# Second attention unit: own buffer for moved x, earlier transpose of routing weights, GpSimd's first weight splits between key products

## The chip, the cores and the metric

The kernel runs on one core of a Trainium2 chip. The metric is the device time of one launch in microseconds; the times shown are of whole launches, and one launch was also profiled. Engines are called by their short names: PE (TensorE), PEld (its weight loads), DVE (VectorE), ACT (ScalarE), POOL (GpSimd), SP (SyncE, which here only issues DMAs).

## The reference, cut to what matters

```python
def _attn_ref(q, k, v, alpha):            # (4, 8, 768, 48)
    for t in range(S):
        state = alpha[:, :, t, :, None] * state + np.einsum('bhd,bhe->bhde', k[:, :, t], v[:, :, t])
        y[:, :, t] = np.einsum('bhd,bhde->bhe', q[:, :, t], state)

def _moe_ref(x, domain_probs, w1, w2):    # N 3072, D 384, E 4, F 1024
    p = domain_probs / (domain_probs.sum(-1, keepdims=True) + 1e-09)
    for e in range(E):
        h = np.maximum(x @ w1[e], 0.0)
        out += p[:, e:e + 1] * (h @ w2[e])

def _moe2_ref(x, w_in, w_out):            # 384 -> 2048 -> 384
    h = x @ w_in
    g = h - np.tanh(h)
    return (g @ w_out).astype(np.float32)

attn_out = _attn_ref(**attn_kwargs)
x = attn_out.transpose(0, 2, 1, 3).reshape(B * S, H * D)
x = _moe_ref(x=x, **moe_kwargs)
return _moe2_ref(x=x, **moe2_kwargs)
```

## The kernel before, in words

**Units and blocks.** The gated attention is computed in twelve units of 256 tokens (three per batch row, each in chunks of 64 tokens). The two dense stages work on six blocks of 512 tokens, two units each. A matmul of the dense stages is done three times, on a rounded high part and a low rest of each operand, which ACT rounds and DVE or POOL subtracts. Block 0 needs units 0 and 1; these two are computed in a prologue, and the other ten are woven into the dense loops, a step of a unit at a time (`units_at`). Units 0 and 1 have two separate sets of tiles; a name with a b at its end (`R2b`, `KUb`, `SCb`) belongs to unit 1.

**The order** on every engine is written out by hand, one stream per engine, and engines wait on semaphores. Ahead of the loop over blocks the streams hold, per unit:

- PE: `diagonal` (L508) and `scores` (L530) are products of keys and queries at three levels; `turn` (L543) transposes the keys; `deltas` (L554) is keys times values of a chunk; `attend` (L567) gives the unit's outputs, in two halves, `attend(u, 0)` and `attend(u, 1)`. In between stands one transpose of the routing weights `prob` (L688). The first product of the dense stage, `first(0, 0)` (L611 to L613), waits for x of both units.
- DVE: `rotate` (L931 to L939, with `distant`, L296 and L300) scales queries for the next level; `pick` (L912) copies wanted scores out of PSUM under a mask from SBUF into `SC`; `states` (L956, L965, L969) carries the state over the four chunks, `state = fade * state + delta`; `probabilities` (L1089 to L1098) normalises the routing weights; `low_x` (L975 to L980) subtracts for the low part of x.
- ACT: `lay` (L751) lays out the turned keys, `join` (L735 to L741) puts scores and queries together, `carry` (L764, L770) copies states next to the values, `high_x` (L779 to L782) rounds x to its high part. Before `carry(0)` ACT copies the transposed routing weights to `PT` (L850).
- POOL: `raise_keys` (L1198) scales the keys, `tabulate` (L1174) makes tables of decay products, `split_low` (L1209) makes the low rest of one slot of weights; `prepare(2)` (L1174, L1184, L296, L300) is unit 2's table and query work.
- SP: loads; then `move(0)` and `move(1)` (L354), six small DMAs each, which bring the rows that `high_x` and `low_x` left in the tile `XS` to their places in the block's x tile `XB`; and behind them the loads of further weights.

**What orders the work near the change.** There is one tile `XS`. `high_x(u)` waits ahead of its first write until all six DMAs of `move(u - 1)` have landed (L778). PE's stream is `scores(1, 2, 1)`, `turn(1, 0)`, `turn(1, 1)`, the transpose of `prob`, `attend(0, 0)`, and so on. ACT's stream there is `join(0)`, the copy to `PT`, `carry(0)`, `lay(1, 0)`, `lay(1, 1)`, `join(1)`, `high_x(0)`, `carry(1)`, `high_x(1)`. `join(1)` waits for all picks of unit 1 and its last `rotate`. DVE's stream there is `probabilities`, `states(0)`, `pick(1, 2, 0)`, `rotate(1, 2)`, `pick(1, 2, 1)`, `states(1)`, `low_x(0)`, `low_x(1)`. POOL's stream has the four first splits behind `raise_keys(1, 2)` and a wait for `rotate(1, 2)`, and `prepare(2)` behind them.

Of the kernel before, what the change touches and what calls it, by code (L numbers as in the profile page):

```python
# [7 lines left out]
fp32 = mybir.dt.float32  # L8
f32r = mybir.dt.float32r
i32 = mybir.dt.int32  # L10
ALU = mybir.AluOpType
ACT = mybir.ActivationFunctionType
# [3 lines left out]
E, DM, F, F2 = 4, 384, 1024, 2048  # L16
N = B * S
P = 128
CH = 64
# [4 lines left out]
SPARE = P // 2 - D  # L24
TB = 512
NTB = N // TB
TT = TB // P
# [4 lines left out]
UT = 256  # L32
# [20 lines left out]
LEAD = 4  # L53
# [32 lines left out]
def own(u):  # L86

    return int(u == 1)
# [6 lines left out]
def turn_of(u):  # L95

    return len(same_set(u))
# [47 lines left out]
def program(nc, qka_d, v_d, dp_d, w1_d, w2_d, win_d, wout_d, mask_d, ones_d, ident_d, out_d):  # L145
    ctx = ExitStack()
    with ctx:
# [5 lines left out]
        def place(name, words, dt=fp32):  # L153
            offset[name] = at[0]
            at[0] += (4 * words + 31) // 32 * 32
            assert at[0] <= nc.sbuf_usable_end, name
            return nc.alloc_sbuf_tensor_at(name, [P, words], dt, offset=offset[name])
# [6 lines left out]
        ident = place("ident", P)  # L164
# [26 lines left out]
        TOTALS = sum(SPAN) // 4 * 5 + sum(SPAN[1:])  # L191
        TOT = [place("TOT", TOTALS), lend("TOTb", TOTALS, "XB1", 2 * KT * TB, UW)]
        T64 = [place(f"T64_{n}", CHUNKS) for n in range(2)]
        XS = place("XS", 2 * UT, f32r)

        scratch_d = nc.dram_tensor("scratch", (SLOTS, P, RW), fp32, kind="Internal").ap()
        probs_d = nc.dram_tensor("probs", (E * NTB * TT, P), fp32, kind="Internal").ap()
# [105 lines left out]
        def fill_bank(u, k):  # L303
            return bank[RING_ALONE * u + k % RING_ALONE] if u < AHEAD else a_bank[k % 2]
# [30 lines left out]
        def _(sp):  # L335
# [12 lines left out]
            def move(u):  # L348
                for j in (2, 0, 1):
                    sp.wait_ge(x_low[own(u)], 3 * turn_of(u) + (2 if j == 2 else 3))  # L350
                    for hh in range(2):
                        src = XS[CH * hh + SPARE * j:CH * hh + SPARE * (j + 1), :].rearrange("p (h t) -> p h t", h=2)
                        dst = x_tile(u)[CH * hh + D:CH * hh + CH, :, j, x_tokens(u)]
                        sp.dma_start(dst.bitcast(fp32), src.bitcast(fp32)).then_inc(moved[own(u)], 16)  # L354

# [116 lines left out]
        def _(pe):  # L472
# [63 lines left out]
            def turn(u, n):  # L536
                if u == 0:
                    pe.wait_ge(ident_in, 16)
                pe.wait_ge(keys_up[own(u)], 3 * turn_of(u) + 3)
                bank_free(u, 14 + n)  # L540
                for m in range(4):
                    c = (4 * n + m) * P
                    last = nc.tensor.transpose(fill_bank(u, 14 + n)[:, m * P:m * P + P], KU[own(u)][:, c:c + P], ident[:, :])  # L543
                last.then_inc(filled[own(u)], 1)
# [137 lines left out]
            deltas(0, 1)  # L682
            scores(1, 2, 0)
            scores(1, 2, 1)
            turn(1, 0)
            turn(1, 1)
            pe.wait_ge(prob_step, E + 2)
            nc.tensor.transpose(bank[3][0:E * NTB * TT, 0:P], prob[:, :], ident[:, :]).then_inc(prob_turned, 1)  # L688
            attend(0, 0)
            pe.wait_ge(prob_laid, 1)  # L690
            attend(0, 1)
# [30 lines left out]
        def _(act):  # L722
# [49 lines left out]
            def high_x(u):  # L772
                x, t = x_tile(u), x_tokens(u)
                if u // 2 >= 2:
                    act.wait_ge(hid, SLOTS * (u // 2 - 1))
                act.wait_ge(filled[own(u)], filled_at(u, 18))
                if u:
                    act.wait_ge(moved[own(u - 1)], 96 * turn_of(u - 1) + 96)  # L778
                nc.scalar.activation(XS[:, 0:UT], fill_bank(u, 18)[:, UT:2 * UT], ACT.Copy).then_inc(x_high[own(u)], 1)  # L779
                nc.scalar.activation(x[:, 0, 2, t], fill_bank(u, 18)[:, 0:UT], ACT.Copy).then_inc(x_high[own(u)], 1)  # L780
                act.wait_ge(filled[own(u)], filled_at(u, 19))
                nc.scalar.activation(x[:, 0, 0:2, t], fill_bank(u, 19)[:, :].rearrange("p (a t) -> p a t", a=2),  # L782
                                     ACT.Copy).then_inc(x_high[own(u)], 1)
# [95 lines left out]
        def _(dve):  # L879
# [92 lines left out]
            def low_x(u):  # L972
                x, t = x_tile(u), x_tokens(u)
                dve.wait_ge(x_high[own(u)], 3 * turn_of(u) + 2)
                nc.vector.tensor_tensor(XS[:, UT:2 * UT], fill_bank(u, 18)[:, UT:2 * UT], XS[:, 0:UT].bitcast(fp32),  # L975
                                        ALU.subtract).then_inc(x_low[own(u)], 1)
                nc.vector.tensor_tensor(x[:, 1, 2, t], fill_bank(u, 18)[:, 0:UT], x[:, 0, 2, t].bitcast(fp32),
                                        ALU.subtract).then_inc(x_low[own(u)], 1)
                dve.wait_ge(x_high[own(u)], 3 * turn_of(u) + 3)
                nc.vector.tensor_tensor(x[:, 1, 0:2, t], fill_bank(u, 19)[:, :].rearrange("p (a t) -> p a t", a=2),  # L980
                                        x[:, 0, 0:2, t].bitcast(fp32), ALU.subtract).then_inc(x_low[own(u)], 1)
# [178 lines left out]
        @block.gpsimd  # L1160
        def _(pool):
            def tabulate(u, first=0, last=9):
                n = 9 * turn_of(u)
                for i in range(first, last):
                    t, two, three = tables(u, i // 3)
                    if i:
                        pool.wait_ge(tabled[own(u)], n + i)
                    if i % 3 == 0:
                        out, a, b = two, t[:, :, 0:3], t[:, :, 1:4]
                    elif i % 3 == 1:  # L1170
                        out, a, b = three, two[:, :, 0:2], t[:, :, 2:4]
                    else:
                        out, a, b = total(u, i // 3 + 1).rearrange("p (n a) -> p n a", a=1), three[:, :, 0:1], t[:, :, 3:4]
                    nc.gpsimd.tensor_tensor(out, a, b, ALU.mult).then_inc(tabled[own(u)], 1)  # L1174

            def prepare(u):
                n = turn_of(u)
                pool.wait_ge(a_in[own(u)], 16 * (n + 1))
                pool.wait_ge(rotated[own(u)], 3 * n)
                pool.wait_ge(keys_up[own(u)], 3 * n)  # L1180
                pool.wait_ge(stated[own(u - 2)], stated_at(u - 2, states_in(u - 2)))
                tabulate(u, 0, 1)
                pool.wait_ge(q_in[own(u)], 16 * (n + 1))
                nc.gpsimd.tensor_tensor(queries(u, 0, 0, 4), R1[own(u)][:, 0:UW].rearrange("p (n b) -> p n b", b=4),  # L1184
                                        tables(u, 0)[0], ALU.mult).then_inc(spread[own(u)], 1)
                pool.wait_ge(spread[own(u)], 2 * n + 1)
                pool.wait_ge(tabled[own(u)], 9 * n + 1)
                distant(nc.gpsimd, u, 0).then_inc(spread[own(u)], 1)
                tabulate(u, 1, 9)

            def raise_keys(u, level):
                h = LEVELS[level]
                pool.wait_ge(filled[own(u)], filled_at(u, 5 + 4 * level))
                pool.wait_ge(tabled[own(u)], 9 * turn_of(u) + 3 * level + 2)
                t, two, three = tables(u, level)
                for sub, x in ((0, three[:, :, 1:2]), (1, two[:, :, 2:3]), (2, t[:, :, 3:4])):
                    k = blocks(KU[own(u)][:, :], h)[:, :, sub, :]
                    last = nc.gpsimd.tensor_tensor(k, k, x.to_broadcast([P, UW // (4 * h), h]), ALU.mult)  # L1198
                last.then_inc(keys_up[own(u)], 1)

            def attention(u, step):
                if step in (3, 6, 9):
                    raise_keys(u, step // 3 - 1)
                if step == 13 and follower(u) is not None:
                    prepare(follower(u))

            def split_low(g):
                pool.wait_ge(w_high, g + 1)
                nc.gpsimd.tensor_tensor(ring_split(g, 1), WS[g % STAGES][:, :].rearrange("p (w c) -> p w c", w=2),  # L1209
                                        ring_split(g, 0).bitcast(fp32), ALU.subtract).then_inc(w_low, 1)  # L1210

            pool.wait_ge(a_in[1], 16)
            tabulate(1, 0, 1)
            raise_keys(0, 0)
            tabulate(1, 1, 9)
            raise_keys(0, 1)
            raise_keys(1, 0)
            raise_keys(0, 2)
            raise_keys(1, 1)
            raise_keys(1, 2)  # L1220
            pool.wait_ge(rotated[1], 3)
            for g in range(LEAD):
                split_low(g)
            prepare(2)
            for m in range(NTB):
                for s in range(SLOTS1):
                    for u, step in units_at(m, s):
                        attention(u, step)
                    if m == 0:
                        split_low(s + LEAD)  # L1230
# [38 lines left out]
```

## Time and profile before

| what | value |
|---|---|
| time, median of 3 runs | 1415.84 us (1415.15 to 1416.24) |
| the profiled execution's own time | 1413.88 us |
| its span, first to last instruction | 1412.0 us |
| busy share of the span: PE / PEld / DVE / ACT / POOL | 96% / 80% / 62% / 40% / 20% |
| mean granted TensorE clock | 0.984 of full speed |
| the same in the first five of 40 slices of the span | 0.9, 0.6, 0.7, 0.9, 0.9 |
| chain that ended last, by engine | PE 87%, DVE 9%, issue 2%, ACT 1%, DMA 1% |

A slice is 35.3 us. PE's busy share is 0.3, 0.5, 0.5 in the first three slices and 0.9 in all later ones. A granted clock of 1.0 is 2.4 GHz, 0.5 is 1.2 GHz.

### The profile page before, as it was taken

How to read it: one execution, taken by the hardware profiler on the slowest of the kernel's cores; microseconds unless marked ns; L12 is line 12 of the kernel's file. 1: busy time of each engine (PE TensorE's matmuls, PEld its weight loads, DVE VectorE, ACT ScalarE, POOL GpSimd, SP SyncE). 2: the span in 40 equal slices, each digit the busy share in tenths (PEclk: the TensorE clock that was granted, in tenths of full speed). 3: DMA queues.
4: the chain of work that ended last, by engine and by line, in shares of the span. 5: the costliest groups of instructions: out<-in, count | busy, mean ns of one | idle time of the engine just before them, and what ended most of it. 6: DMA issues, size and time to landing. Idle time of an engine off the chain costs nothing.

```text
span 1412.0 us, 25677 instructions
## 1 busy us (share of the span) xinstructions
PE 1352.7 (96%) x10177; PEld 1133.5 (80%) x10177; DVE 877.8 (62%) x1676; ACT 561.2 (40%) x1004; POOL 281.1 (20%) x277
## 2 busy tenths in 40 slices
PE   3559999999999999999999999999999999999999
PEld 3447878887878898888898787888787889888888
DVE  9856574896465686554587455487546468423386
ACT  1414325861313662222474321475131366211175
POOL 4645766001313001304000312300131000000000
PEclk9679999999999999999999999999999999999999
DMA  7258697976565655655655665565656465655552
GB/s 218 69 188 294 220 304 249 335 276 209 175 209 198 236 185 177 221 186 197 224 209 167 227 203 187 194 235 180 209 176 194 167 214 187 209 193 193 181 201 88
DMA packets 104966, 289.06 MB, mean 205 GB/s; under 512 B 10032, under 2 KB 64912, under 8 KB 104848
## 3 DMA queue, kind: packets, MB, share of 16 engines
q1 hardware_dynamic: 104848, 287.43, 60.3%
q8 instruction: 81, 1.33, 0.4%
q14 instruction: 37, 0.30, 0.1%
HBM read 242.52 MB, written 42.52 MB: 202 GB/s over the span
## 4 chain that ended last, share of the span: by engine, by line
PE 87%; DVE 9%; issue 2%; ACT 1%; DMA 1%; SPq 0%; DVEq 0%; ACTq 0%
PE bank L611 14%; PE bank L612 13%; PE bank L613 13%; PE bank L635 9%; PE bank L637 9%; PE bank L636 9%; PE bank L661 4%; PE bank L659 4%; PE bank L660 4%; PE bank L530 3%; PE bank L567 2%; PE bank L554 1%; DVE SC L912 1%; PE bank L508 1%; PE bank L543 1%
## 5 line engine op out<-in xcount | busy, mean ns | idle before, releaser
L809 ACT ACTIVATE HH<-GG 128x512 fp32r<-128x512 f32 x192 | 121.2, 631 | 664.4 <-PE bank L637 529.5
L611 PE MATMUL bank<-XB,RG 128*128 128x512 f32 x864 | 349.6, 405 | 10.1 <-DMA XB<-XS 9.8
L612 PE MATMUL bank<-XB,RG 128*128 128x512 f32 x864 | 340.2, 394 | 0.0
L613 PE MATMUL bank<-XB,RG 128*128 128x512 f32 x864 | 339.2, 393 | 0.0
L1013 DVE SCALAR_TENSOR_TENSOR GG<-bank,PB 128x512 f32<-128x512 f32 x192 | 133.3, 694 | 326.0 <-PE bank L613 325.7
L635 PE MATMUL bank<-HH,RG 128*128 128x512 f32 x576 | 224.7, 390 | 1.5 <-ACT OUT L842 1.5
L636 PE MATMUL bank<-HH,RG 128*128 128x512 f32 x576 | 224.3, 389 | 0.0
L637 PE MATMUL bank<-HL,RG 128*128 128x512 f32 x576 | 224.2, 389 | 0.0
L1198 POOL TENSOR_TENSOR KU<-KU,TOT 128x256 f32<-128x256 f32 x88 | 68.9, 809 | 704.2 <-PE bank L530 704.2
L611 PEld LDWEIGHTS bank<-XB,RG 128*128 128x128 f32 x864 | 162.7, 188 | 50.9 <-issue 10.1
L613 PEld LDWEIGHTS bank<-XB,RG 128*128 128x128 f32 x864 | 162.7, 188 | 35.6
L612 PEld LDWEIGHTS bank<-XB,RG 128*128 128x128 f32 x864 | 162.9, 189 | 28.8
L1019 DVE TENSOR_TENSOR HL<-GG,HH 128x512 fp32r<-128x512 f32 x192 | 157.8, 822 | 8.8 <-ACT HH L809 8.8
L912 DVE COPY_PREDICATED SC<-masks,bank 128x192 f32<-128x192 int32 (+2 forms) x396 | 99.1, 358 | 69.5 <-PE bank L530 69.3
L661 PE MATMUL bank<-RG,HL 128*128 128x384 f32 x384 | 129.5, 337 | 0.0
L659 PE MATMUL bank<-RG,HH 128*128 128x384 f32 x384 | 129.3, 337 | 0.0
L635 PEld LDWEIGHTS bank<-HH,RG 128*128 128x128 f32 x576 | 108.1, 188 | 26.3 <-issue 3.6
L660 PE MATMUL bank<-RG,HH 128*128 128x384 f32 x384 | 128.9, 336 | 0.0
L637 PEld LDWEIGHTS bank<-HL,RG 128*128 128x128 f32 x576 | 108.1, 188 | 22.8
L636 PEld LDWEIGHTS bank<-HH,RG 128*128 128x128 f32 x576 | 108.1, 188 | 22.5
L1036 DVE TENSOR_TENSOR GG<-SQ,bank 128x512 f32<-128x512 f32 x96 | 65.6, 683 | 39.2 <-ACT TH L819 39.2
L818 ACT ACTIVATE SQ<-bank 128x512 f32<-128x512 f32 x96 | 57.2, 596 | 67.6 <-PE bank L613 67.6
(127 smaller groups left out, 1684.1 us busy)
## 6 DMA issues: line engine op xcount, KB each, us to landing
RG<-scratch SPq DMA_DIRECT2D x240, 768.0 KB, 4.3
scratch<-RG SPq DMA_DIRECT2D x48, 768.0 KB, 5.1
VS<-vp SPq DMA_DIRECT2D x11, 768.0 KB, 5.9
WS<-w SPq DMA_DIRECT2D x32, 192.0 KB, 3.3
PB<-probs SPq DMA_DIRECT2D x6, 1024.0 KB, 7.2
AU<-qka SPq DMA_DIRECT2D x11, 512.0 KB, 5.4
R<-qka SPq DMA_DIRECT2D x11, 512.0 KB, 5.3
KU<-qka SPq DMA_DIRECT2D x11, 512.0 KB, 5.8
```

The source lines that it names most:

```text
L611: nc.tensor.matmul(out, w1(g, 0, kt), x_part(m, 0, kt), start=(kt == 0), stop=False)
L612: nc.tensor.matmul(out, w1(g, 0, kt), x_part(m, 1, kt), start=False, stop=False)
L613: last = nc.tensor.matmul(out, w1(g, 1, kt), x_part(m, 0, kt), start=False, stop=(kt == KT - 1))
L635: nc.tensor.matmul(out, w2(g, 0)[:, c], HH[:, h_slot(g)], start=(s == 0), stop=False)
L636: nc.tensor.matmul(out, w2(g, 1)[:, c], HH[:, h_slot(g)], start=False, stop=False)
L637: return nc.tensor.matmul(out, w2(g, 0)[:, c], HL[:, h_slot(g)], start=False, stop=(s == SLOTS1 - 1))
L659: nc.tensor.matmul(out, HH[:, h], w2(g, 0), start=(f == 0), stop=False)
L660: nc.tensor.matmul(out, HH[:, h], w2(g, 1), start=False, stop=False)
L661: last = nc.tensor.matmul(out, HL[:, h], w2(g, 0), start=False, stop=(f == SLOTS2 - 1))
L809: nc.scalar.activation(HH[:, h_slot(g)], GG[:, h_slot(g)], ACT.Copy).then_inc(high, 1)
L1013: nc.vector.scalar_tensor_tensor(GG[:, h_slot(g)], h_bank[s % 2][:, :], 0.0, PB[:, e * TB:e * TB + TB], op0=ALU.max, op1=ALU.mult).then_in ...
L1019: nc.vector.tensor_tensor(HL[:, h_slot(g)], GG[:, h_slot(g)], HH[:, h_slot(g)].bitcast(fp32), ALU.subtract).then_inc(low, 1)
```

## The change

`XS` becomes a pair of tiles, one per set, so that unit 1 writes `XSb`; the wait ahead of `high_x` is now for the last move out of the same tile, which unit 1 has none of. On PE the transpose of `prob`, with its wait for `probabilities`, goes ahead of `turn(1, 0)`. On POOL the first two splits go ahead of `raise_keys(1, 1)`, behind a wait for the first `queries_up` of unit 1 (which `rotate(1, 0)` gives), the third stands between `raise_keys(1, 1)` and `raise_keys(1, 2)`, the fourth behind it; the wait for `rotate(1, 2)` is gone.

```diff
-        XS = place("XS", 2 * UT, f32r)
+        XS = [place("XS", 2 * UT, f32r), place("XSb", 2 * UT, f32r)]
...
-                        src = XS[CH * hh + SPARE * j:CH * hh + SPARE * (j + 1), :].rearrange("p (h t) -> p h t", h=2)
+                        src = XS[own(u)][CH * hh + SPARE * j:CH * hh + SPARE * (j + 1), :].rearrange("p (h t) -> p h t", h=2)
...
             scores(1, 2, 1)
+            pe.wait_ge(prob_step, E + 2)
+            nc.tensor.transpose(bank[3][0:E * NTB * TT, 0:P], prob[:, :], ident[:, :]).then_inc(prob_turned, 1)
             turn(1, 0)
             turn(1, 1)
-            pe.wait_ge(prob_step, E + 2)
-            nc.tensor.transpose(bank[3][0:E * NTB * TT, 0:P], prob[:, :], ident[:, :]).then_inc(prob_turned, 1)
             attend(0, 0)
...
                 act.wait_ge(filled[own(u)], filled_at(u, 18))
-                if u:
-                    act.wait_ge(moved[own(u - 1)], 96 * turn_of(u - 1) + 96)
-                nc.scalar.activation(XS[:, 0:UT], fill_bank(u, 18)[:, UT:2 * UT], ACT.Copy).then_inc(x_high[own(u)], 1)
+                if turn_of(u):
+                    act.wait_ge(moved[own(u)], 96 * turn_of(u))
+                nc.scalar.activation(XS[own(u)][:, 0:UT], fill_bank(u, 18)[:, UT:2 * UT], ACT.Copy).then_inc(x_high[own(u)], 1)
...
-                nc.vector.tensor_tensor(XS[:, UT:2 * UT], fill_bank(u, 18)[:, UT:2 * UT], XS[:, 0:UT].bitcast(fp32),
+                nc.vector.tensor_tensor(XS[own(u)][:, UT:2 * UT], fill_bank(u, 18)[:, UT:2 * UT], XS[own(u)][:, 0:UT].bitcast(fp32),
...
             raise_keys(0, 2)
+            pool.wait_ge(queries_up[1], 1)
+            split_low(0)
+            split_low(1)
             raise_keys(1, 1)
+            split_low(2)
             raise_keys(1, 2)
-            pool.wait_ge(rotated[1], 3)
-            for g in range(LEAD):
-                split_low(g)
+            split_low(3)
             prepare(2)
```

PE's order in the prologue, from `deltas` of unit 0 to the first `attend`: a piece of the difference between the two streams (L530 is `scores`, L543 `turn`, L686 or L688 the transpose of `prob`).

```order
 L554 MATMUL bank<-VS,KJ 48x48 x32
 L530 MATMUL bank<-R2b,KUb 64x96 x32
+L686 MATMUL bank<-ident,prob 96x128
 L543 MATMUL bank<-ident,KUb 128x128 x8
-L688 MATMUL bank<-ident,prob 96x128
 L567 MATMUL bank<-R_85,VS 48x64
```

The one transpose of `prob` now stands ahead of unit 1's eight key transposes, with its wait; nothing else on PE moved.

POOL's order in the prologue, from unit 1's level 0 keys to the start of `prepare(2)` (L1198 is `raise_keys`, L1209 `split_low`, L1174 with `TOT<-AU` the first of `prepare(2)`).

```order
 L1198 TENSOR_TENSOR KUb<-KUb,AUb 128x256
 L1198 TENSOR_TENSOR KU<-KU,TOT 128x16x16 x3
+L1209 TENSOR_TENSOR RG_57<-WS_65,RG_57 128x2x384
+L1209 TENSOR_TENSOR RG_58<-WS_66,RG_58 128x2x384
 L1198 TENSOR_TENSOR KUb<-KUb,TOTb 128x64x4 x3
+L1209 TENSOR_TENSOR RG_59<-WS_67,RG_59 128x2x384
 L1198 TENSOR_TENSOR KUb<-KUb,TOTb 128x16x16 x3
-L1209 TENSOR_TENSOR RG_57<-WS_65,RG_57 128x2x384
-L1209 TENSOR_TENSOR RG_58<-WS_66,RG_58 128x2x384
-L1209 TENSOR_TENSOR RG_59<-WS_67,RG_59 128x2x384
 L1209 TENSOR_TENSOR RG_60<-WS_68,RG_60 128x2x384
 L1174 TENSOR_TENSOR TOT<-AU 128x768
```

Three of the four splits moved ahead; the fourth and `prepare(2)` follow `raise_keys(1, 2)` at once. The instructions of DVE, ACT and SP keep their order; those of unit 1 name `XSb` in place of `XS`.

## Rows read from the trace of the kernel before

**Rows 1.** Busy time by stretch, with granted clock, DMA share and GB/s last.

```profile
84.50:110.00 25.50, 21.59 (x222) 16.72 (x223) 19.59 (x34) 5.46 (x8) 10.93 (x7) 0.86 0.85 285
...
200.00:1400.00 1200.00, 1197.42 (x8364) 1004.38 (x8363) 730.28 (x1372) 492.64 (x885) 169.92 (x180) 1.00 0.61 205
```

**Rows 2.** Chain of waits in the prologue: start, length, what.

```profile
56.51 1.94 PE bank L543 x8
...
75.77 1.99 DMA XB<-XS
...
82.50 1.96 DMA XB<-XS
84.59 0.76 PE bank L611
85.35 0.43 PE bank L612
...
102.45 0.23 PE bank L613
```

**Rows 3.** Timeline of ACT: start, length, instruction, [idle before <- releaser].

```profile
58.70 0.27 ACT L850 ACTIVATE PT<-bank 96x128 f32<-96x128 f32 x1 [7.59 <-PE bank L688]
...
59.77 1.39 ACT L770 ACTIVATE VS<-ST 48x576 f32<-48x576 f32 x2
61.06 2.75 ACT L751 ACTIVATE KJb<-bank 64x192 f32<-64x192 f32 x8
63.84 1.28 ACT L735 ACTIVATE QBb<-SCb 64x512 f32<-64x512 f32 x2
...
67.55 0.38 ACT L779 ACTIVATE XS<-bank 128x256 fp32r<-128x256 f32 x1
...
77.85 0.39 ACT L779 ACTIVATE XS<-bank 128x256 fp32r<-128x256 f32 x1 [6.98 <-DMA XB<-XS]
```

**Rows 4.** Timeline of PE at the two ends of attend(1, 0).

```profile
71.26 0.27 PE L567 MATMUL bank<-R2b,VSb 128*48 128x64 f32 x1 [5.01 <-issue]
...
72.90 0.31 PE L567 MATMUL bank<-QBb,VSb 128*48 128x64 f32 x1
```

**Rows 5.** Timeline of SP: first DMA of move(0) and of move(1).

```profile
71.62 0.74 SPq L354 DMA_DIRECT2D XB<-XS  x1
...
79.33 0.58 SPq L354 DMA_DIRECT2D XB<-XS  x1
```

**Rows 6.** Timeline of DVE, 39 to 59 us.

```profile
39.75 0.41 DVE L300 TENSOR_TENSOR R1b<-R1b,TOTb 128x256 f32<-128x256 f32 x1
...
46.63 2.07 DVE L939 TENSOR_TENSOR R<-R,TOT 128x256 f32<-128x256 f32 x3
...
52.40 0.26 DVE L1098 TENSOR_TENSOR prob<-prob,small 128x96 f32<-128x96 f32 x1
...
54.17 0.35 DVE L969 TENSOR_TENSOR ST<-ST,bank 112x192 f32<-112x192 f32 x1
...
56.41 1.09 DVE L939 TENSOR_TENSOR R2b<-R2b,TOTb 128x256 f32<-128x256 f32 x3
57.42 1.28 DVE L912 COPY_PREDICATED SCb<-masks,bank 128x192 f32<-128x192 int32 x6
```

**Rows 7.** Timeline of POOL, 46 to 60 us.

```profile
46.64 2.65 POOL L1198 TENSOR_TENSOR KUb<-KUb,TOTb 128x256 f32<-128x256 f32 x3 [7.36 <-PE bank L530]
52.45 2.18 POOL L1198 TENSOR_TENSOR KUb<-KUb,TOTb 128x256 f32<-128x256 f32 x3 [3.17 <-PE bank L530]
...
57.58 1.81 POOL L1209 TENSOR_TENSOR RG<-WS,RG 128x768 fp32r<-128x768 f32 x1 [2.94 <-DVE R2b L939]
```

**Rows 8.** Timeline of POOL in prepare(2), 64 to 71 us.

```profile
64.78 1.47 POOL L1174 TENSOR_TENSOR TOT<-AU 128x768 f32<-128x768 f32 x1
66.20 2.46 POOL L1184 TENSOR_TENSOR R<-R,AU 128x1024 f32<-128x1024 f32 x1
68.74 1.58 POOL L296 TENSOR_TENSOR R<-R,AU 128x512 f32<-128x512 f32 x1
```

**Rows 9.** Timeline of DVE beside it, a fade of states(1).

```profile
66.88 2.00 DVE L965 TENSOR_TENSOR ST<-ST,T 112x192 f32<-112x192 f32 x1
```

## The prediction

> **What bounds the kernel now.** I read the busy time by stretch first. From 200 to 1400 us PE works 1197.42 of 1200 us at a granted clock of 1.00 [rows 1]: no edit to the prologue changes that part, and PE does the same work there after the change. So the question is only by how much the first product of the dense stage, which starts at 84.59 us [rows 2], moves, and whether what lies behind it moves with it. The view for that is the chain of waits up to there, and then the timelines of the engines that it names.
>
> Backwards from 84.59: the last DMA of `move(1)` is issued at 82.50 and lands 1.96 us later [rows 2]. Its first is issued at 79.33 [rows 5], so from the first issue to the first product it takes 84.59 - 79.33 = 5.26 us. The six issues follow each other without a gap: SP's issuing is what limits them. They could start because ACT wrote `XS` for unit 1 at 77.85, after an idle wait of 6.98 us that a DMA ended [rows 3]: the last of `move(0)`, issued at 75.77 and landed at 77.76 [rows 2]. From ACT's write to the first issue it is 79.33 - 77.85 = 1.48 us (two roundings, two subtractions). The data for that write were there long before: `attend(1, 0)` ran from 71.26 and ended at 72.90 + 0.31 = 73.21 [rows 4]. And `attend(1, 0)` waited for ACT: ACT works in one unbroken row of instructions from 58.70, the copy to `PT`, through `carry(0)`, `lay(1)` at 61.06, `join(1)` at 63.84, `high_x(0)` at 67.55 and `carry(1)` [rows 3]. Before 58.70 it sat idle for 7.59 us, until the transpose of `prob` [rows 3], which stands on PE behind `turn(1)`, 56.51 to 58.45 [rows 2].
>
> **Edit 1, the transpose of `prob` ahead of `turn(1)`.** Its input is ready at 52.40 + 0.26 = 52.66 [rows 6]. PE has nothing to do then: `turn(1)` cannot start before 56.51, so the wait that now stands ahead of it holds nobody up; this cover is 3.8 us, and only if `probabilities` came that much later would `turn(1)` pay. I put the transpose at 52.7 and the `PT` copy at 53.2 (the matmul is one of the size that `turn` does eight of in 1.94 us). The copies of the state began 59.77 - 58.70 = 1.07 us behind `PT` [rows 3] and would now begin at 54.3, but the third state is there only at 54.17 + 0.35 = 54.52 [rows 6]; 1.39 us from there is 55.95 in place of 61.16. So `attend(0)` starts behind `turn(1)`, at about 58.5. `lay(1)`, 2.75 us in eight copies [rows 3], starts when the first half of `turn(1)` is done, about 57.6, and ends at 60.35 in place of 63.81. ACT could then start `join(1)` 3.5 us earlier than before.
>
> **Edit 2, the splits.** POOL sits idle from the end of `raise_keys(0, 2)` to 46.64, 7.36 us [rows 7]. The new wait is met at 39.75 + 0.41 = 40.16 [rows 6]; two splits of 1.81 us [rows 7] end at 43.8, before `raise_keys(1, 1)` can start. It ends at 46.64 + 2.65 = 49.29, and the third split fills 49.3 to 51.1, before 52.45. So no key product on PE is later. DVE works in these gaps on picks, and the rows say these do not mind POOL: six picks took 1.28 us [rows 6] beside a split that began at 57.58 [rows 7]. Cost of the first three: nothing, covered by POOL's idle time.
>
> The fourth split and `prepare(2)` are another matter. `raise_keys(1, 2)` ends at 52.45 + 2.18 = 54.63 [rows 7], so the split runs to about 56.5, and `prepare(2)` follows with instructions of 1.47, 2.46 and 1.58 us [rows 8], 8 us earlier than before. On DVE `rotate(1, 2)` stands at 56.41, 3 instructions in 1.09 us with POOL idle [rows 6]. The wait that is taken out kept just this apart. What it costs is read from the same three instructions of unit 0: 2.07 us [rows 6] beside three of POOL's in 2.65 us [rows 7]: each, from the second on, finishes only when the POOL instruction under way has ended. A fade of 112x192 took 2.00 us beside POOL's 2.46 [rows 8, 9]. Hence: the first of the three passes behind the split (56.9), the second waits for the 1.47 us instruction (58.4), the third for the 2.46 us one (61.0), and six picks follow, 1.28 us: `pick(1, 2, 1)` ends at 62.3 in place of 58.70. The bounds are 58.70 (no hold) and 63.5 (the 1.47 us instruction gets in ahead of the first, and the third waits for the 1.58 us one too). I take 62.3, which goes by the pattern of the rows at 46.6, where DVE's first one went ahead.
>
> The Trainium skill (page "SBUF — State Buffer", section "Who interferes with whom") has this as a rule: a VectorE instruction with two SBUF inputs and a GpSimd one that reads SBUF exclude each other for a whole instruction, and who comes first goes first. By its summary, one is to put the engine that is off the critical path behind; this change does the reverse at `rotate(1, 2)`. What it would give if POOL came first is the second case below.
>
> **The sum.** `join(1)` starts at 62.3, when the picks are done, not at 60.35, when ACT is free: 1.54 us earlier than 63.84. So edit 1 gives 3.5 us and edit 2 takes 1.95 of it back. `high_x(0)`, `carry(1)` and `attend(1, 0)` follow as before, 1.54 us earlier: `attend(1, 0)` ends at 71.67. DVE is not late for that: from 62.3 four fades of about 0.8, four additions of 0.35 and 0.75 of `low_x(0)` give 67.7.
>
> **Edit 3, the buffer.** `high_x(1)` now starts when `attend(1, 0)` ends: at 71.7, not 77.85. It was held from 73.21 to 77.85, 4.64 us, and all of this goes. SP must be free: `move(0)` now starts at 67.7; from its first issue to its last it was 75.77 - 71.62 = 4.15 us [rows 2, 5], and with the last one's 0.6 it is done at 72.5. `move(1)` can start at 71.7 + 1.48 = 73.2, so SP is in time by 0.7 us; if DVE were late by more than that, the line of twelve issues would be the next bound. The first product comes at 73.2 + 5.26 = 78.44. Check: 84.59 - 78.44 = 6.15 = 1.54 + 4.64, but for rounding. Behind it, weight loads on SP follow `move(1)` directly, and DVE, ACT and PE start on data, so the stretch from there on moves as a whole. The later moves use `XS` alone as before, amid 1197.42 us of PE work, and gain nothing.
>
> The profiled execution took 1413.88 us, which would become 1407.7. The median of the runs shown is 1415.84, 1.96 above it; against it the forecast is 1415.84 - 6.15 = **1409.7 us**.
>
> **Rivals.**
> - *POOL first at `rotate(1, 2)`.* Picks end at 63.5, and `join(1)` starts only 0.3 us earlier than before: gain 0.3 + 4.64 = 5.0 us, 1410.9. For it: POOL and DVE arrive within 0.1 us of each other at 56.4. Against: at 46.6 they did too, and DVE passed. This is the rule's "who comes first", and only the trace after can tell. Chance 0.20.
> - *No hold.* `join(1)` starts at 60.35, and then SP's twelve issues bound it: `low_x(0)` about 67.4, gain about 7, 1408.8. Against it speak the 2.07 us at 46.63 [rows 6]. Chance 0.08.
> - *The clock.* The first product ran at the lower level (1.2 GHz), 0.43 us a matmul against 0.23 later [rows 2], behind idle PE: `attend(1, 0)` ended at 73.21 [rows 4], and its like `attend(1, 1)`, 1.6 to 1.9 us, at about 75, so for 9.6 us. Now it is idle for about 5. If it is still granted full speed, nine matmuls save 9 x 0.2 = 1.8 more: 1407.9. Against: `attend(1, 0)` also began slow (0.31 us a piece) after 5.01 us idle [rows 4]. Chance 0.06.
> - *Given back in the first block.* From 84.5 to 110 PE is idle for 3.9 us and the clock is 0.86 [rows 1]. A different phase there could drop the clock for two more products of nine, 3.6 us, which leaves 2.5: 1413.3. For it: DVE, POOL and DMA (share 0.85) are all busy there. Against: all that starts there starts from the same events. Chance 0.10.
> - *Slower: picks are held by the splits.* If a masked copy had to wait as a two-input one does, the four splits and `prepare(2)` would sit on DVE's chain from 40.2 on: at most 4 x 1.81 + 1.47 + 2.46 + 1.58 = 12.75 us, less the 6.15: 1422.4. It decides from 6.15 + 2.8 = 9 us of holds on. Against: the picks at 57.42 beside the split at 57.58 [rows 6, 7], unchanged; those read PSUM and one tile of SBUF. Chance 0.04.
>
> **How the numbers follow.** The forecast has 0.52, POOL first 0.20, no hold 0.08, the clock 0.06, together 0.86, all faster by more than 0.2% (2.8 us, about what a measurement of this kernel can tell from no change). Given back is the 0.10 within it, held picks the 0.04 of slower. The range goes from 1407.4 (the clock case, 1407.9, less half a microsecond for the scatter of the runs, 1415.15 to 1416.24) to 1413.0, the edge of 0.2%; what is left out are the last two cases, 0.14.
>
> **What the new profile would show.** Right: the copy to `PT` near 53.2; splits near 40.2, 42.0, 49.3 and 54.6; three L939 of unit 1 near 56.4 that take about 4.6 us together in place of 1.09; ACT's write of `XSb` with no DMA as its releaser; twelve L354 issues with hardly a gap; the first L611 near 78.4; PE 1197 of 1200 us busy later on. Wrong: picks (L912) of more than 0.3 us each beside splits; `turn(1)` later than 56.6; a first L611 at 78.4 with a span that is not about 6 us shorter.

## The result, and the profile after

| | before | after |
|---|---|---|
| median | 1416.04 us (4 runs, 1415.15 to 1416.57) | 1408.78 us (4 runs, 1407.92 to 1408.89) |
| ratio | | 0.9947, 95% interval 0.9935 to 0.9960 |
| profiled execution, time and span | 1413.88, 1412.0 us | 1408.89, 1407.1 us |
| start of the first dense product (L611) | 84.59 us | 78.45 us |

The medians differ by 7.3 us. The forecast was 6.15 us less and 1409.7 us, in a range of 1407.4 to 1413.0. The first product starts at 78.45 us where 78.44 was forecast; that this agrees to 0.01 us is luck (see the sum below).

The timeline of ACT after the change, the columns as in [rows 3]:

```profile
53.14 0.27 ACT L850 ACTIVATE PT<-bank 96x128 f32<-96x128 f32 x1 [1.95 <-PE bank L686]
...
54.63 1.39 ACT L770 ACTIVATE VS<-ST 48x576 f32<-48x576 f32 x2 [0.45 <-DVE ST L969]
57.71 2.76 ACT L751 ACTIVATE KJb<-bank 64x192 f32<-64x192 f32 x8 [1.69 <-PE bank L543]
62.29 1.28 ACT L735 ACTIVATE QBb<-SCb 64x512 f32<-64x512 f32 x2 [1.82 <-DVE SCb L912]
...
65.99 0.38 ACT L779 ACTIVATE XS<-bank 128x256 fp32r<-128x256 f32 x1
...
71.41 0.38 ACT L779 ACTIVATE XSb<-bank 128x256 fp32r<-128x256 f32 x1 [2.08 <-PE bank L567]
```

The copy to `PT` comes at 53.14 instead of 58.70. ACT's unbroken row of [rows 3] now has a gap: it is free at 60.47 (57.71 + 2.76) and waits 1.82 us for DVE's picks before `join(1)`. Its write of `XSb` waits for PE's `attend(1, 0)` and no longer for a DMA.

The timeline of DVE after the change, beside [rows 6]:

```profile
56.49 4.58 DVE L939 TENSOR_TENSOR R2b<-R2b,TOTb 128x256 f32<-128x256 f32 x3
60.99 1.27 DVE L912 COPY_PREDICATED SCb<-masks,bank 128x192 f32<-128x192 int32 x6
62.17 0.55 DVE L965 TENSOR_TENSOR ST<-ST,T 112x192 f32<-112x192 f32 x1
63.30 0.35 DVE L969 TENSOR_TENSOR ST<-ST,bank 112x192 f32<-112x192 f32 x1 [0.58 <-PE bank L554]
63.69 1.52 DVE L965 TENSOR_TENSOR ST<-ST,T 112x192 f32<-112x192 f32 x1
...
67.34 0.42 DVE L975 TENSOR_TENSOR XS<-bank,XS 128x256 fp32r<-128x256 f32 x1
```

And the timeline of POOL over the same time, beside [rows 7, 8]:

```profile
40.30 3.60 POOL L1209 TENSOR_TENSOR RG<-WS,RG 128x768 fp32r<-128x768 f32 x2 [0.96 <-DVE R1b L300]
46.73 2.64 POOL L1198 TENSOR_TENSOR KUb<-KUb,TOTb 128x256 f32<-128x256 f32 x3 [2.83 <-PE bank L530]
49.33 1.83 POOL L1209 TENSOR_TENSOR RG<-WS,RG 128x768 fp32r<-128x768 f32 x1
52.54 2.17 POOL L1198 TENSOR_TENSOR KUb<-KUb,TOTb 128x256 f32<-128x256 f32 x3 [1.38 <-PE bank L530]
54.67 1.99 POOL L1209 TENSOR_TENSOR RG<-WS,RG 128x768 fp32r<-128x768 f32 x1
56.63 1.64 POOL L1174 TENSOR_TENSOR TOT<-AU 128x768 f32<-128x768 f32 x1
58.24 2.54 POOL L1184 TENSOR_TENSOR R<-R,AU 128x1024 f32<-128x1024 f32 x1
```

The reader is to see two things. Three L939 take 4.58 us in place of 1.09; they end in step with POOL's instructions (58.27, 60.78). The six picks take 1.27 us as before. And the splits sit in POOL's gaps as meant; the `raise_keys` after them begin 0.09 us later than before (46.73 and 52.54 against 46.64 and 52.45), where unit 1's key transposes on PE are 0.07 us later too.

The timeline of SP after the change, beside [rows 5]:

```profile
68.11 4.70 SPq L354 DMA_DIRECT2D XB<-XS  x6
72.88 4.07 SPq L354 DMA_DIRECT2D XB<-XSb  x6
77.00 0.58 SPq L386 DMA_DIRECT2D WS<-w  x1
```

The last links of the chain of waits after the change, beside [rows 2]:

```profile
65.34 0.64 ACT R2b L741
65.98 3.44 issue
69.42 3.67 PE bank L567 x64
...
73.11 0.60 ACT XB L782
...
73.74 0.70 DVE XB L980
...
74.46 0.58 SPq L354
...
76.36 1.96 DMA XB<-XSb
...
78.45 0.76 PE bank L611
```

The landing of `move(0)` is gone from the chain. In its place stands `attend(1, 1)`, the second half of the 64 products in the row of L567, with the last rounding and subtraction.

**Where the profiled spans part from the medians.** The first product came 6.14 us earlier, yet the profiled span is shorter by only 4.9. The missing 1.24 us lie behind the first product. Busy time by stretch, columns as in [rows 1]; the change:

```profile
78.40:82.20 3.80, 3.75 (x13) 2.76 (x17) 0.00 (x0) 0.00 (x0) 0.00 (x0) 0.59 0.68 233
94.00:98.50 4.50, 4.50 (x14) 3.53 (x12) 2.20 (x7) 0.23 (x1) 4.20 (x4) 0.50 0.89 325
```

The kernel before, the same places counted from its first product:

```profile
84.50:88.30 3.80, 3.71 (x9) 2.81 (x9) 0.00 (x0) 0.00 (x0) 0.00 (x0) 0.51 0.72 232
100.10:104.60 4.50, 4.50 (x24) 3.47 (x20) 3.16 (x9) 0.99 (x2) 3.90 (x4) 0.81 0.91 318
```

In both kernels PE is idle for 3.8 us from some 10.3 us after the first product on. Behind that stretch it ran 4.5 us at a granted clock of 0.50 (1.2 GHz) in the change and at a mean of 0.81 in the kernel before. In the first 25 us, 15 dense matmuls of 512 columns started 0.43 us apart in the change's profile, and 9 before. Six times 0.2 us is the 1.2. The same kernel profiled again (second group of experiments) had 9.

### The profile page after: what moved, and what is told of

Same layout as the page of the kernel before. It is cut to its first block, busy times and chain, and to the rows that moved or that the text cites. A ratio compares the mean times of both kernels' runs of the same rounds, so it can differ in the third digit from the quotient of the medians.

```text
span 1407.1 us, 25676 instructions
## 1 busy us (share of the span) xinstructions
PE 1353.9 (96%) x10177; PEld 1134.0 (81%) x10177; DVE 877.8 (62%) x1676; ACT 561.2 (40%) x1004; POOL 280.8 (20%) x277
## 4 chain that ended last, share of the span: by engine, by line
PE 87%; DVE 8%; issue 2%; ACT 1%; DMA 0%; SPq 0%; DVEq 0%; ACTq 0%
PE bank L611 14%; PE bank L612 13%; PE bank L613 13%; PE bank L635 9%; PE bank L636 9%; PE bank L637 9%; PE bank L661 4%; PE bank L659 4%; PE bank L660 4%; PE bank L530 3%; PE bank L567 2%; PE bank L554 1%; DVE SC L912 1%; PE bank L508 1%; DVE RG L1070 1%
## 5 line engine op out<-in xcount | busy, mean ns | idle before, releaser
L611 PE MATMUL bank<-XB,RG 128*128 128x512 f32 x864 | 350.2, 405 | 5.7 <-DMA XB<-XSb 5.4
L1198 POOL TENSOR_TENSOR KU<-KU,TOT 128x256 f32<-128x256 f32 x88 | 68.6, 806 | 704.4 <-PE bank L530 704.4
L611 PEld LDWEIGHTS bank<-XB,RG 128*128 128x128 f32 x864 | 163.0, 189 | 46.8 <-issue 5.8
L912 DVE COPY_PREDICATED SC<-masks,bank 128x192 f32<-128x192 int32 (+2 forms) x396 | 99.0, 357 | 69.8 <-PE bank L530 69.5
```

Of the source, the lines that this page charges most:

```text
L611: nc.tensor.matmul(out, w1(g, 0, kt), x_part(m, 0, kt), start=(kt == 0), stop=False)
```

## The experiments

Each profile starts its prologue a little differently: unit 1's key transposes (L543), which no edit moves, began anywhere from 56.5 to 58.0 us. So the start of the first product is given twice, as read, and counted as if L543 had begun at 56.51. "Slow" is the number of dense matmuls 0.43 us apart behind it. The last column is the median against the median of before on the same chip. A to D are the theories that each expectation names.

| kernel | L543 | first L611 | counted | slow | span less first L611 | median, less before |
|---|---|---|---|---|---|---|
| before | 56.51 | 84.59 | 84.59 | 9 | 1327.4 | |
| change | 56.59 | 78.45 | 78.4 | 15 | 1328.7 | 1408.78, -7.3 |
| change, second time | 57.05 | 78.92 | 78.4 | 9 | 1327.6 | 1408.85, -6.8 |
| edit 3 alone | 57.87 | 84.18 | 82.8 | 15 | 1328.8 | 1412.78, -3.2 |
| edit 1 alone | 56.60 | 82.33 | 82.2 | 8 | 1327.4 | 1412.42, -3.5 |
| edit 2 alone | 57.96 | 83.46 | 82.0 | 9 | 1327.6 | 1413.29, -2.7 |
| without edit 2 | 57.23 | 80.06 | 79.3 | 15 | 1328.6 | 1408.79, -7.2 |
| without edit 3 | 57.72 | 82.26 | 81.1 | 12 | 1327.9 | 1411.05, -5.0 |
| prepare(2) waits | 57.24 | 78.64 | 77.9 | 11 | 1328.0 | 1408.35, -7.3 |
| ACT issues half of move(1) | 57.02 | 77.90 | 77.4 | 7 | 1327.6 | 1407.45, -8.2 |
| the last two together | 56.48 | 75.55 | 75.6 | 14 | 1328.1 | 1406.77, -8.9 |
| high_x(0) early | 57.78 | 79.48 | 78.2 | 10 | 1327.8 | 1408.97, -6.4 |
| high_x(0) early, ACT issues | 56.86 | 76.93 | 76.6 | 15 | 1327.8 | 1406.27, -9.1 |
| waits, ACT issues half of both | 56.81 | 75.83 | 75.5 | 15 | 1328.0 | 1406.01, -9.3 |

The whole times of one kernel scatter by 0.5 to 4 us (edit 3 alone: 1410.67 to 1414.82 in 11 runs). The profiles show two sources: the start of the prologue, and the slow matmuls. The count of these does not settle the last stretch alone: the two last rows have 15 and yet only 1327.8 and 1328.0 us, with an idle stretch of 3.2 and 3.0 us in place of 3.8. So a mechanism is judged by the counted start, and the medians only say whether it reaches the end; the 95% intervals of their ratios reach 1.3 to 2.0 us to each side. But all kernels except the change have one profile only, and a counted start holds luck of its own: `move(0)`'s six issues on SP take 3.9 to 5.0 us, as one of them is long or not (last section). Differences under 0.8 us are therefore read together with these issues. The last column and the counted gain agree to 1.5 us in every row but one (without edit 2, 5.3 counted and 7.2 by a median of five runs that fell into 1408.7 and 1411).

### One edit at a time

**Edit 3 alone**: the second tile `XSb`, neither order touched.

```diff
-        XS = place("XS", 2 * UT, f32r)
+        XS = [place("XS", 2 * UT, f32r), place("XSb", 2 * UT, f32r)]
```

> Edit 3 alone (XSb), nothing else. Theory A (ACT, SP and DVE are three chains that bound in turn, so the edits do not add up): with move(0) still starting at 71.6 us, SP's twelve issues follow each other, move(1) begins near 76.4 and the first product (L611) at 81.7 us, 2.9 us earlier than the 84.59 of before. Theory B (the prediction's ledger, in which each edit has its own price): the wait of 4.64 us goes, first product near 80.0. Whole time down by 2.9 (A) or 4.6 us (B).

Counted, the first product came at 82.8: 1.8 us earlier, against 2.9 (A) and 4.6 (B). In the median 3.2 us less (ratio 0.9978, 0.9969 to 0.9987). SP went from `move(0)` to `move(1)` in 4.95 us without a wait, as A has it; the missing 1.1 us lie ahead of it: `move(0)` began at 73.96 - 1.36 = 72.6 and not at 71.6, half of that because the deltas of unit 1 were done 0.56 us later (PE took 5.55 us for `attend(0, 0)`, `attend(0, 1)` and these deltas at a mean granted clock of 0.61, and 5.00 us at 0.70 in the kernel before), half because POOL held the fades longer (2.18, 1.23 and 0.68 us against 0.42, 2.00 and 1.23). B is out.

**Edit 1 alone**: the transpose of `prob` ahead of `turn(1, 0)`.

```diff
+            pe.wait_ge(prob_step, E + 2)
+            nc.tensor.transpose(bank[3][0:E * NTB * TT, 0:P], prob[:, :], ident[:, :]).then_inc(prob_turned, 1)
             turn(1, 0)
             turn(1, 1)
```

> Edit 1 alone. Theory A: join(1) starts at 60.4 instead of 63.84, but states(1) is held by the last split and by prepare(2), low_x(0) ends near 70.0, and high_x(1) still waits for move(0): first product near 83.0 us, 1.6 us earlier. Theory B: 3.5 us earlier, near 81.1.

First product at 82.2, 2.4 us earlier (A: 83.0). Of this, 0.8 is luck: none of `move(0)`'s issues took over 0.75 us here, where one took 1.41 before. `move(0)` itself began at 70.1 counted, 1.5 us earlier, as A has it (1.6). `join(1)` began 3.3 us earlier, at 60.52, but not all of that came through: the fades stand in the way. Timeline of DVE in this run:

```profile
58.70 1.00 DVE L965 TENSOR_TENSOR ST<-ST,T 112x192 f32<-112x192 f32 x1
...
63.10 2.02 DVE L965 TENSOR_TENSOR ST<-ST,T 112x192 f32<-112x192 f32 x1
...
65.55 1.12 DVE L965 TENSOR_TENSOR ST<-ST,T 112x192 f32<-112x192 f32 x1
...
67.09 2.00 DVE L965 TENSOR_TENSOR ST<-ST,T 112x192 f32<-112x192 f32 x1
...
69.40 0.42 DVE L975 TENSOR_TENSOR XS<-bank,XS 128x256 fp32r<-128x256 f32 x1
```

Four fades take 6.1 us where 1.4 would do (0.36 each). The last three, 5.1 us, stand ahead of `low_x(0)`.

**Edit 2 alone**: the order of POOL as in the change, nothing else.

```diff
+            pool.wait_ge(queries_up[1], 1)
+            split_low(0)
+            split_low(1)
             raise_keys(1, 1)
+            split_low(2)
             raise_keys(1, 2)
-            pool.wait_ge(rotated[1], 3)
-            for g in range(LEAD):
-                split_low(g)
+            split_low(3)
             prepare(2)
```

> Edit 2 alone. Theory A: the three L939 are held and the picks end near 62.3, which ACT's own row (join(1) at 63.84) hides; and with prepare(2) 8 us earlier the fades of states(1) are held less, so low_x(0) comes near 69.4 instead of 71.6: first product near 82.3 us, 2.3 us earlier. Theory B: the edit can only cost, 0 to 2 us later, first product at 84.6 or later.

First product at 82.0 (A: 82.3), 2.6 us earlier. Here too a part is luck: the longest of `move(0)`'s issues took 0.95 us, and its last DMA landed 5.68 us after its first issue, against 6.14 before. `move(0)` began at 69.5 counted, 2.1 us earlier. The timeline of DVE in this run, which began 1.45 us late, shows both sides of the edit:

```profile
57.85 4.55 DVE L939 TENSOR_TENSOR R2b<-R2b,TOTb 128x256 f32<-128x256 f32 x3
63.52 0.56 DVE L965 TENSOR_TENSOR ST<-ST,T 112x192 f32<-112x192 f32 x1
...
67.93 0.36 DVE L965 TENSOR_TENSOR ST<-ST,T 112x192 f32<-112x192 f32 x1
...
68.71 0.36 DVE L965 TENSOR_TENSOR ST<-ST,T 112x192 f32<-112x192 f32 x1
...
69.49 0.37 DVE L965 TENSOR_TENSOR ST<-ST,T 112x192 f32<-112x192 f32 x1
```

The L939 are held (4.55 us), which ACT's row hides here; and with POOL's long instructions over before `states(1)` comes, three of the four fades take 0.36 us and not up to 2.00 [rows 9]. The edit is a gain by itself.

**The change without edit 2** (edits 1 and 3, POOL's order as before):

> The change without edit 2 (edits 1 and 3). Theory A: picks end at 58.7 and join(1) starts at 60.4, but the fades of states(1) wait for the splits and prepare(2) again; low_x(0) near 70.0, SP's twelve issues from there, first product near 80.1 us, 1.6 us later than the 78.45 of the change. Theory B: edit 2 takes 1.95 us, so without it the first product comes near 77.5, 1 us earlier than with the change.

First product at 79.3, 0.9 us later than with edit 2, where B had it 1 us earlier. The direction is A's, the size 0.7 us less. What is missing is seen in SP's timeline of this run:

```profile
70.79 3.96 SPq L354 DMA_DIRECT2D XB<-XS  x6
74.79 0.59 SPq L354 DMA_DIRECT2D XB<-XSb  x1
```

`move(0)` took 74.79 - 70.79 = 4.00 us to the first issue of `move(1)`, against 72.88 - 68.11 = 4.77 in the change. One of its six issues took 1.38 us there, and none over 0.75 here. With the long one it would be 80.1, as expected. The median, 1408.79, does not tell the kernel from the change.

**The change without edit 3** (edits 1 and 2, one `XS`, its wait as before):

> The change without edit 3: edits 1 and 2 with the one tile XS. Theory A: move(0) starts at 68.0 as in the change, its last DMA lands 6.1 us later at 74.2, high_x(1) follows and the first product comes 6.74 us behind its write, at 81.0 (counted with unit 1's key transposes at 56.51); edit 3 is then worth 2.6 us on top of the other two. Theory B: edit 3 is worth the 4.64 us that ACT waited for it in the kernel before: first product near 83.0.

First product at 81.1, by A to 0.1 us. In this run's timeline ACT waits for `move(0)` to land:

```profile
75.52 0.38 ACT L779 ACTIVATE XS<-bank 128x256 fp32r<-128x256 f32 x1 [5.07 <-DMA XB<-XS]
```

So the buffer is worth 2.7 us on top of the other two (81.1 less 78.4), 1.8 alone. The sum of the three alone is 1.8 + 2.4 + 2.6 = 6.8, and together they give 6.2. But 0.8 and 0.5 of this sum are the short issues of `move(0)` in the runs of edit 1 and edit 2; without them it is about 5.5, and whether the three add up to more or less than the bundle is not shown.

### What bounds the change

**prepare(2) waits for rotate(1, 2)**:

```diff
             split_low(3)
+            pool.wait_ge(rotated[1], 3)
             prepare(2)
```

> The change, with one wait put back: POOL waits for rotate(1, 2) between its fourth split and prepare(2). Theory A (the hold of the three L939 behind prepare(2) costs what lies between ACT's 60.4 and the picks' 62.3, and then SP's twelve issues bind): three L939 take 1.1 us again, picks end at 58.8, join(1) starts at 60.5, low_x(0) is done near 67.1, first product near 77.1 us, 1.3 us earlier than the 78.45 of the change. Theory C (the hold is hidden, since states(1) has to wait for deltas(1) and for POOL anyway): first product 78.2 or later.

Less than half of what A said: 77.9, 0.5 us earlier. The L939 were fast again (1.1 us) and `join(1)` began at 60.4 counted, but the fades were held for 1.03 and 1.05 us and `move(0)` began at 68.0, as in the change. From there SP's twelve issues follow each other to the last:

```profile
68.73 4.61 SPq L354 DMA_DIRECT2D XB<-XS  x6
73.38 3.77 SPq L354 DMA_DIRECT2D XB<-XSb  x6
```

The long one among `move(0)`'s issues took 1.27 us here, 1.38 in the change's first profile and 1.71 in its second. With an issue as long as those, this kernel would come at 78.0 to 78.4, so the gain of the wait alone in this run is between nothing and 0.4 us. In the run with both edits below the same fades took 0.52 and 0.68 and `move(0)` began at 67.1. Half of that 1 us are the fades; the other half came ahead of them: `attend(0, 0)` and `attend(0, 1)`, ahead of unit 1's deltas, took 3.57 us here and 3.09 there. In the first 3.15 us of them PE was granted 0.50 of its clock here, and 0.59 there.

**The change again**:

> The changed kernel itself on the same chip as its neighbours: first product near 78.4 us; the time from there to the end of the span is 1327.5 us where 8 or 9 of the 512-column matmuls in the first 20 us run at the lower clock, and 1328.7 where 15 do (both were seen). Against before: 5 to 7 us less.

78.4 counted, as in the first profile, with 9 slow matmuls in place of 15, and 1327.6 us behind it in place of 1328.7. The same 78.4 has another last link, though. SP in this run:

```profile
68.57 5.04 SPq L354 DMA_DIRECT2D XB<-XS  x6
73.65 3.77 SPq L354 DMA_DIRECT2D XB<-XSb  x6
```

One of `move(0)`'s issues took 1.71 us, so `move(1)` began later and its six issues followed each other without a wait (3.77 us), where in the first profile they took 4.07 with a wait for the last subtraction. The two bounds, SP's issues and `attend(1, 1)`, lie within 0.4 us of each other.

**ACT issues half of move(1)**:

```diff
-                    for hh in range(2):
+                    for hh in range(1 if u == 1 else 2):
...
             high_x(1)
+            for j in (2, 0, 1):
+                act.wait_ge(x_low[1], 2 if j == 2 else 3)
+                src = XS[1][CH + SPARE * j:CH + SPARE * (j + 1), :].rearrange("p (h t) -> p h t", h=2)
+                dst = x_tile(1)[CH + D:2 * CH, :, j, x_tokens(1)]
+                act.dma_start(dst.bitcast(fp32), src.bitcast(fp32)).then_inc(moved[1], 16)
```

> The change, with three of the six DMAs of move(1) issued from ACT, which is idle there. Theory A (the issue rate of one queue bounds the last link): SP issues two DMAs less after x_low(1) is complete at 74.4, first product near 77.2 us, 1.25 us earlier. Theory D (the transfers themselves, about 2 us from issue to landing, or a shared issuing path bind): no gain, 78.4.

77.4, 1.0 us earlier, against A's 77.2 and D's 78.4: A. `move(0)` began at 68.0 counted as in the change, and its issues took no less time (4.95 us to the first of `move(1)`), so this gain is not luck. The transfers do not bind, the issues of one queue do.

**Both**:

> Both of the last two edits on top of the change: prepare(2) waits for rotate(1, 2), and ACT issues half of move(1). Theory A: x_low(1) is complete near 72.6, two more issues on each queue, first product near 75.3 us, 3.1 us earlier than the change, about 1405.7 us in all. If the two gains do not add, near 77.1.

75.6 against 75.3: 2.8 us earlier than the change, more than the 0.5 and 1.0 of the two alone. Each had left the other's bound in place. Of the difference, 1 us is that `move(0)` began at 67.1 here (and in the last run below) and at 68.0 where `prepare(2)` waited alone, which ACT's issues have no part in.

**high_x(0) ahead of join(1)**, on ACT, and then the same with ACT's issues:

```diff
-            join(1)
             high_x(0)
+            join(1)
             carry(1)
```

> The change with high_x(0) ahead of join(1) on ACT, in the 1.8 us in which ACT waits for the picks. carry(1) and attend(1, 0) come 1.15 us earlier (68.3 instead of 69.4). Theory A (SP's twelve issues bind as soon as ACT's row is shorter by 0.3 us): with low_x(0) unmoved and move(0) still starting at 68.0, the first product (counted with unit 1's key transposes at 56.51) comes at 78.1, only 0.3 us earlier than the 78.38 of the change. Theory B (each link's gain counts in full): 77.2.

> The same with three DMAs of move(1) on ACT, so that SP's queue no longer binds. Theory A: now the 1.15 us count: first product near 76.2, 1.2 us earlier than the 77.39 of the run with ACT's issues alone, and 1.9 earlier than with high_x(0) early alone. Theory B: about the same, 76.2; the two differ in the run above.

78.2 and 76.6, so A in the first and 0.4 us less than expected in the second. The first says the most: `attend(1, 0)` begins 0.7 us earlier counted (68.67, 69.34 in the change; less than the expected 1.15, since the end of `high_x(0)` waits for `attend(0, 1)` and moves `join(1)` to 62.7), and 0.2 of it arrive. SP in that run:

```profile
69.30 4.87 SPq L354 DMA_DIRECT2D XB<-XS  x6
74.21 3.77 SPq L354 DMA_DIRECT2D XB<-XSb  x6
78.03 0.58 SPq L386 DMA_DIRECT2D WS<-w  x1
```

Twelve issues without a gap from the end of `low_x(0)` on. With three of them on ACT the first product comes 1.6 us earlier than that, at 76.6 (expected 76.2), and 0.8 earlier than with ACT's issues alone: now the shorter row of ACT counts.

**Half of both moves on ACT, prepare(2) waiting**:

> The version with prepare(2) waiting and ACT issuing half of move(1), and with half of move(0) on ACT too. SP is then never the bound; what is left are attend(1, 1), a rounding, a subtraction, two issues and a landing: first product near 75.2, 0.4 us earlier than the 75.58 without it, about 1406.3 us in all. If ACT's three issues come late and push high_x(1) back, 75.6 or later.

ACT's three issues of `move(0)` stand between `carry(1)` and `high_x(1)`, those of `move(1)` behind `high_x(1)`. 75.5: next to nothing over 75.6, against the 0.4 expected. Timelines of ACT's and of SP's queue in this run:

```profile
67.36 2.03 ACTq L790 DMA_DIRECT2D XB<-XS  x3
...
71.46 0.60 ACT L782 ACTIVATE XB<-bank 128x512 fp32r<-128x512 f32 x1 [1.05 <-PE bank L567]
71.46 2.84 ACTq L790 DMA_DIRECT2D XB<-XSb  x3
```

```profile
67.36 2.31 SPq L354 DMA_DIRECT2D XB<-XS  x3
71.23 2.81 SPq L354 DMA_DIRECT2D XB<-XSb  x3
```

ACT's three issues did not push `high_x(1)` back (`XSb` was written at 69.75), and both queues began at once. But from the last issue to the first product it took 75.83 - 73.45 = 2.38 us, against 75.55 - 73.46 = 2.09 in the run of "Both": the last DMA was one of ACT's, whose issue took 0.86 us and which landed 2.25 us after it began. The last issue itself came 0.35 us earlier counted, so the landing took back what the issues gave. The bound has moved to `attend(1, 1)` and what follows it. By its median of 1406.01 us (ratio to before 0.9936, 0.9922 to 0.9949) this is the fastest version, 2.8 us under the change; it cannot be told from its two neighbours at 1406.27 and 1406.77.

## Why the prediction was right, and which of its steps was not

- **Edit 1.** Forecast: `PT` at 53.2, the copies of the state at 54.5, `attend(0)` at 58.5, ACT free at 60.35. Measured: 53.14, 54.63, 58.46, 60.47. `turn(1)` was not held up. Right.
- **The splits in POOL's gaps.** Forecast near 40.2, 42.0, 49.3 and 54.6; measured 40.30, 42.1, 49.33, 54.67, and no pick is longer: the rival of held picks is out.
- **The hold of rotate(1, 2).** Forecast ends at 56.9, 58.4 and 61.0 and 4.6 us for the three; measured 4.58, the picks ending at 62.26 (forecast 62.3). DVE's first went ahead of POOL, so the rival of "POOL first" did not come to pass, in this profile or in the second, where `join(1)` began at 62.2 counted, nor in the five others with this order on POOL (4.55 to 4.58 us for the three). Here the trace agrees with the Trainium skill (page "SBUF — State Buffer", section "Who interferes with whom"): the one waits for the whole of the other's instruction. The second and third L939 ended 0.3 us behind POOL's at 58.27 and 60.78.
- **The sum.** `join(1)` forecast at 62.3, `attend(1, 0)` ending at 71.67, `XSb` written at 71.7, `move(1)` at 73.2, first product at 78.44. Measured: 62.29, 71.4, 71.41, 72.88, 78.45. That the number came out to 0.01 us is luck, for two errors cancel: `move(1)` began 0.3 us early, and the 5.26 us from there to the first product, which the prediction took over from before, were 5.57. SP had to wait for `x_low(1)` once more, 74.10 to 74.46, since `attend(1, 1)` ended at 73.09 only and a rounding and a subtraction follow it; in the trace before all of `attend(1, 1)` was over long before `move(1)`. `move(0)` was forecast at 67.7 and began at 68.11. Its 4.15 us from the first issue to the last, also taken from before, came again as 4.11, with one long issue in both; without one it is 3.3 to 3.4 us (edit 1 alone, without edit 2). And 73.2 + 5.26 is 78.46, not 78.44: the terms are rounded.
- **What was wrong: the ledger.** The prediction wrote that edit 1 gives 3.5 us, that "edit 2 takes 1.95 of it back", and that of the 4.64 us at the buffer "all of this goes". The total was computed along the new chain and stands; the shares do not. Edit 2 gives 2.6 us alone (2.1 with SP's issues as before) and 0.9 on top of the other two (1.7, were SP's long issue there in both runs). The step that failed compared `join(1)` with and without the hold and left DVE's `states(1)` as it was, though [rows 9] already showed a fade held for 2.00 us by `prepare(2)`: without edit 2 that stays, and `low_x(0)` comes late. And the buffer is worth 2.7 us, not 4.64, because the other two edits let `move(0)` start and land 3.5 us earlier even without it (ACT's write of `XS` at 74.3 counted, not 77.85), and with it SP cannot issue `move(1)` before `move(0)` is out.
- **The clock.** The rival of a faster first product did not come true: its first matmuls still ran 0.43 us apart, six of them in the change's first profile, seven in its second and in the kernel before. The rival "given back in the first block" came true by a third of its price in the profiled execution, 1.2 of 3.6 us, and is no property of the change: the second profile did not have it. It is why the span is shorter by 4.9 us where the first product came 6.1 us earlier. By the prediction's own list this was a sign of being wrong ("a span that is not about 6 us shorter"); the second profile's span was 5.5 us shorter, its prologue having begun 0.5 us late.
- **The last 1.1 us.** The medians moved by 7.3 us and the first product by 6.1 to 6.2; the second set of runs gave 6.8. The 95% interval of the ratio, 0.9935 to 0.9960, is 5.7 to 9.2 us, so the 6.15 lies within it. The profiled execution of the kernel before was itself fast (1413.88; the medians of before were 1415.35 to 1416.04). No profile of a slower execution of before was taken, so where those lose their 2 us was not shown.

## What to carry to other kernels

Price a bundle of edits along the chain that will exist afterwards, and do not hand each edit the wait that it removes in the old trace: three chains (ACT's row, DVE's fades beside POOL, SP's twelve issues) were within about 1 us of each other here, and each edit alone met the next one. Small DMAs whose issue takes 0.6 us each are a chain of their own when a dozen follow each other ahead of the first product; three of the twelve on a queue that is idle gave 1.0 us alone, and 2.3 us (77.9 to 75.6) once `prepare(2)` waited as well, of which 1 us is `move(0)`'s earlier start and not theirs. When a term of the sum is taken over from the old trace, ask what it did not have to wait for there: the 5.26 us held no wait for `attend(1, 1)`. Work that is moved earlier on GpSimd can cost VectorE at the new place and free it at the old one; count both.

## What the runs showed of the hardware that was not expected

- One of `move(0)`'s issues on SP took 1.25 to 1.71 us against the usual 0.59 in ten of the fourteen profiles, at the second to the fifth place; in the other four none took over 0.95. This DMA and the one issued just ahead of it landed 2.6 to 3.2 us after issue, the others mostly after 1.95 to 2.0. Where SP's issues bind, that is 0.7 to 1.1 us on the first product. What causes it was not tried.
- The last DMA of `move(1)` issued from ACT landed 2.23 to 2.25 us after issue in three of the four runs where ACT issued half (2.00 in "Both"), against 1.94 to 2.00 for the last ones on SP. In the last run this 0.3 us is what kept a further 0.35 us of earlier issues from paying; why ACT's took longer was not tried.
- The same kernel, with the same start of the dense stage, ran 9 or 15 matmuls at the lower clock level in its first 25 us, 1.1 us of difference in the span. The medians of the kernel before lay between 1415.35 and 1416.04 us in five sets of runs, and the 95% intervals of the ratios reach up to 2.0 us to each side; an effect of 1 us is better read from one event in the trace, and even that needs more than one profile.
